# Expert steps of a token-routed kernel: gathered rows are turned in the middle of a step's low parts, each half of the next weights is loaded when its own buffer is free, and the state rows' ranks stand ahead of their gates

## What is computed

```python
def _moe_ref(x, w_in, w_out):            # 4352 rows of 512, hidden 2048
    h = x @ w_in
    g = np.maximum(0.01 * h, h)
    return g @ w_out

def _moe2_ref(x, w_gate, w_output_gate, w1, w2):     # 8 experts, hidden 1024
    logits = x @ w_gate
    e_idx = np.argmax(logits, axis=1)
    probs = softmax(logits);  gate_w = probs[arange(N), e_idx]
    eom = sigmoid(x @ w_output_gate)
    for e in range(E):
        mask = e_idx == e
        h = np.maximum(x[mask] @ w1[e], 0.0)
        out[mask] = gate_w[mask, None] * eom[mask, e, None] * (h @ w2[e])
```

## Time and profile before

| | us |
|---|---|
| median of 3 runs | 1158.08 |
| lowest and highest | 1157.42 and 1158.69 |
| the profiled execution | 1158.76 |
| its span in the trace | 1157.0 |
| PE busy | 1114.1 (96%) |
| DVE busy | 632.6 (55%) |
| ACT busy | 405.8 (35%) |
| POOL busy | 275.6 (24%) |

### The profile page before, as it was taken

One profiled execution on the slowest core, in us unless ns is written; L12 is line 12 of the kernel. 1 busy time (PEld: TensorE's weight loads), 2 busy tenths in 40 slices (PEclk: granted clock), 3 DMA queues, 4 the chain that ended last, 5 costly groups with the idle time before them and its releaser, 6 DMA issues.

```text
span 1157.0 us, 18341 instructions
## 1 busy us (share of the span) xinstructions
PE 1114.1 (96%) x6530; PEld 903.9 (78%) x6531; DVE 632.6 (55%) x1421; ACT 405.8 (35%) x754; POOL 275.6 (24%) x337
## 2 busy tenths in 40 slices
PE   5999999999999999999999999999999999888995
PEld 2777777777777777777777888889899989678884
DVE  6684574764854746747554577553433436366342
ACT  4344334434433443344343553321211214244211
POOL 1000001010010010000100203554455365655643
PEclk8999999999999999999999999999999999999998
DMA  9311120120210201200102411761111124443211
GB/s 346 125 45 37 37 78 1 42 73 1 76 40 18 80 19 37 79 1 1 37 1 75 126 38 48 201 195 55 39 48 59 37 56 98 144 105 107 55 39 35
DMA packets 41054, 79.01 MB, mean 68 GB/s; under 512 B 11398, under 2 KB 13190, under 8 KB 40967
## 3 DMA queue, kind: packets, MB, share of 16 engines
q1 hardware_dynamic: 29957, 53.48, 15.2%
q0 software_dynamic: 11040, 24.77, 7.5%
HBM read 60.31 MB, written 20.61 MB: 70 GB/s over the span
## 4 chain that ended last, share of the span: by engine, by line
PE 80%; DVE 6%; issue 4%; DMA 4%; POOL 2%; ACT 1%; POOLq 1%; SPq 0%; DVEq 0%; ACTq 0%
PE bank L529 25%; PE bank L531 24%; PE bank L530 24%; PE bank L562 3%; DMA raw<-w_dram 2%; POOL xq L438 2%; DMA xq<-rows_dram,part_now 2%; PE bank L580 1%; PE bank L596 1%; DVE w_lo L1338 1%; PE bank L604 1%; PE bank L540 1%; PE bank L569 1%; DVE g_buf L1213 0%; DVE o_buf L1600 0%
## 5 line engine op out<-in xcount | busy, mean ns | idle before, releaser
L529 PE MATMUL bank<-wout_lo,gT_hi 128*128 128x512 f32 x544 | 216.0, 397 | 0.0
L531 PE MATMUL bank<-wout_hi,gT_hi 128*128 128x512 f32 x544 | 212.7, 391 | 0.0
L530 PE MATMUL bank<-wout_hi,gT_lo 128*128 128x512 f32 x544 | 212.2, 390 | 0.0
L438 POOL DMA_INDIRECT xq<-rows_dram,part_now x160 | 170.5, 1066 | 69.4 <-issue 54.7
L423 POOL DMA_INDIRECT slots_dram<-tok_i,pos_i x34 | 34.4, 1010 | 616.3 <-DVE pos_i L1313 608.6
L1213 DVE TENSOR_TENSOR g_buf<-g_buf,bank 128x512 f32<-128x512 f32 (+1 forms) x144 | 94.3, 655 | 107.2 <-ACT g_buf L963 106.9
L529 PE MATMUL bank<-xgT_lo,w_hi 128*128 128x256 f32 x512 | 146.3, 286 | 6.0 <-DVE hT_lo L1469 4.7
L530 PE MATMUL bank<-xgT_hi,w_lo 128*128 128x256 f32 x512 | 145.6, 284 | 0.0
L531 PE MATMUL bank<-xgT_hi,w_hi 128*128 128x256 f32 x512 | 145.5, 284 | 0.0
L963 ACT ACTIVATE g_buf<-bank 128x512 f32<-128x512 f32 (+1 forms) x144 | 82.5, 573 | 151.7 <-PE bank L531 150.2
L1217 DVE TENSOR_TENSOR gT_lo<-g_buf,gT_hi 128x512 fp32r<-128x512 f32 (+1 forms) x144 | 95.4, 662 | 72.9 <-ACT gT_hi L969 71.4
(11 more groups left out here) (227 smaller groups left out, 1764.0 us busy)
## 6 DMA issues: line engine op xcount, KB each, us to landing
raw<-w_dram SPq DMA_DIRECT2D x20, 512.0 KB, 8.9
raw<-w_dram SPq DMA_DIRECT2D x10, 1024.0 KB, 14.5
rows_dram<-y_buf SPq DMA_DIRECT2D x8, 1032.0 KB, 4.5
X<-x_in_dram SPq DMA_DIRECT2D x8, 1024.0 KB, 5.5
XT<-xT_in_dram SPq DMA_DIRECT2D x7, 1024.0 KB, 5.7
win<-w_in_dram SPq DMA_DIRECT2D x4, 1024.0 KB, 11.6
y_buf<-w_out_dram POOLq DMA_DIRECT2D x6, 512.0 KB, 7.2
xq<-rows_dram,part_now POOLq DMA_INDIRECT x160
```

What stands on the lines that cost most here:

```text
L438: pool.indirect_dma_start(out=xq[:, 4 * u + a, :], out_offset=None, in_=quarters_dram, in_offset=bass.IndirectOffsetOnAxis(ap=part_now[:, ...
L529: pe.matmul(o, l_hi, r_lo, start=first, stop=False)
L530: pe.matmul(o, l_lo, r_hi, start=False, stop=False)
L531: return pe.matmul(o, l_hi, r_hi, start=False, stop=last)
```

## The change

Five edits.

1. In a step of two tiles DVE does `turn_quarters(i + 1)` behind `h_lo(i, 4)`, ahead of the last three.
2. SP loads `w1` of the next expert when pieces 0 to 3 of the last weights are split, and `w2` when all eight are.
3. The state rows' ranks on PE stand one `f` earlier; on DVE ranks and slots come ahead of the gates, of which only the sum stays in front.
4. `row_now` is written ahead of `plan_order`.
5. The eight stores of 32 state rows each become two of 128.

```diff
@@ SP
-            def load_expert(ex, between=None):
-                load_w1(ex)
-                if between is not None:
-                    sp.wait_ge(gathered, between)
-                load_w2(ex)
@@
             for t in range(2):
-                for q in range(4):
-                    first = (S + NS) * (4 * t + q) + S
-                    sp.dma_start(rows_dram[first:first + NS, :], y_buf[NS * q:NS * q + NS, t, :]).then_inc(y_stored, 16)
+                sp.dma_start(rows_dram.rearrange("(b s) n -> b s n", b=B)[4 * t:4 * t + 4, S:, :], y_buf[:, t, :]).then_inc(y_stored, 16)
@@ load_planned
+                w1_splits = 8 * v - DC if isinstance(v, int) else sp.snap(8 * v - DC)
                 with sp.If(c0 < c1):
                     sp.wait_ge(ctl_ready, 1)
+                    sp.wait_ge(e_lo_done, w1_splits)
+                    load_w1(expert)
+                    if between is not None:
+                        sp.wait_ge(gathered, between)
                     sp.wait_ge(e_lo_done, splits)
-                    load_expert(expert, between)
+                    load_w2(expert)
@@ POOL gather_step, and ACT ahead of its loop
-                pool.wait_ge(y_stored, 16 * (B + 8))
+                pool.wait_ge(y_stored, 16 * (B + 2))
@@ PE first_step_and_last_routing
                     if f == 2:
                         pe.wait_ge(lg_copied, B + 1)
-                    elif f == 3:
                         ranks(B, 2, rank_bank=oacc[0])
@@ DVE: route_gate loses its first instruction to sum_gates
+            def sum_gates(r, tiles):
+                step = Steps(dve, route_step, RS * r + 6, 1)
+                dve.wait_ge(edif_ready, r + 1)
+                step(dve.reduce_sum(gate[:, 0:T], edif[:, 0:T, :], AX.X))
@@ DVE, written-out stretch
             h_lo(0, 0)
-            route_gate(B, 2)
-            route_ranks(B, 2, rank_bank=oacc[0])
+            sum_gates(B, 2)
+            route_ranks(B, 2, rank_bank=oacc[0], after=7)
+            route_slots(B, 2, state=True, after=7)
             h_lo(0, 1)
-            route_slots(B, 2, state=True)
+            route_gate(B, 2, after=7 + 2 + 6)
             h_lo(0, 2)
@@
-            plan_order()
             dve.wait_ge(second_in, 16)
             dve.tensor_scalar(row_now[:, :], second_tok[:, :], NT - 1, None, ALU.min).then_inc(rows_copied, 2)
+            plan_order()
@@ DVE expert_step
                 if tiles == 2:
-                    for f in range(F2):
+                    for f in range(5):
                         h_lo(i, f)
                     turn_quarters(i + 1)
+                    for f in range(5, F2):
+                        h_lo(i, f)
```

More of the change, by code:

```diff
@@ L1096, in _ @@
             act.wait_ge(ctl_ready, 1)
-            act.wait_ge(y_stored, 16 * (B + 8))
+            act.wait_ge(y_stored, 16 * (B + 2))
             with act.Fori(0, E // 2) as w:
@@ L1262, in route, with route_gate @@
                 step.end()
-            def route_gate(r, tiles):
+            def sum_gates(r, tiles):
                 T = tiles
-                step = Steps(dve, route_step, RS * r + 6, 5)
+                step = Steps(dve, route_step, RS * r + 6, 1)
                 dve.wait_ge(edif_ready, r + 1)
                 step(dve.reduce_sum(gate[:, 0:T], edif[:, 0:T, :], AX.X))
+                step.end()
+            def route_gate(r, tiles, after=7):
+                T = tiles
+                step = Steps(dve, route_step, RS * r + after, 4)
                 step(dve.tensor_scalar(gate[:, 0:T], gate[:, 0:T], 1e-9, None, ALU.add))
@@ L1279, in route_gate, with route_ranks @@
                                   ez[:, 0:T].rearrange("p (t q n) -> p t q n", q=1, n=1).broadcast_to([P, T, DC, 1]), ALU.mult).then_inc(gate_ready, 1)
-            def route_ranks(r, tiles, rank_bank=aux[0]):
+            def route_ranks(r, tiles, rank_bank=aux[0], after=11):
                 T = tiles
                 dve.wait_ge(rank_ps, r + 1)
-                step = Steps(dve, route_step, RS * r + 11, T)
+                step = Steps(dve, route_step, RS * r + after, T)
                 for t in range(T):
@@ L1290, in route_ranks, with route_slots @@
                 step.end()
-            def route_slots(r, tiles, state=False):
+            def route_slots(r, tiles, state=False, after=11):
                 T = tiles
-                step = Steps(dve, route_step, RS * r + 11 + T, RS - 11 - T)
+                step = Steps(dve, route_step, RS * r + after + T, 6 if state else 7)
                 dve.wait_ge(rank_read, r + 2)
@@ L1316, in route_slots @@
                     step(dve.tensor_scalar(tokf[:, 0:T], tokf[:, 0:T], float(S + NS), None, ALU.add))
-                    step.end()
+                step.end()
             w8_row = const[0:1, C_W8:C_W8 + E]
@@ L1385, in layer @@
                         if f == 11:
+                            sum_gates(r, 4)
                             route_gate(r, 4)
```

## The result

| | us | |
|---|---|---|
| before | 1157.75 (1157.11 to 1158.69, 4 runs) | profiled execution 1158.76, span 1157.0 |
| after | 1167.16 (1165.79 to 1168.72, 4 runs) | profiled execution 1165.79, span 1164.0 |
| ratio | 1.0081, interval 1.0064 to 1.0098 | forecast 1156.3 (1152.0 to 1162.0) |

The changed kernel is slower by 0.8% on this chip. Sign and range of the forecast were wrong. The medians are 9.4 apart and the two traces 7.0: the profiled execution before was slower than its four timed ones, the one after was the fastest of its four.

What follows compares the result with a forecast made beforehand. PE, busy 80% of the span, was taken as the bound, changeable only through its gaps. Steps 1 and 2 with their lead +2.5, 11 to 14 -2.3, 15 to 18 -2.0: -1.8 in all, giving 1156.3 us (1152.0 to 1162.0).

Steps and rivals of the forecast that it cites:

- term of -2.07: PE's gap ahead of flip_rows(1), waiting for the rows of step 1: edits 3 and 4 remove it, -2.07 us.
- Rival C: Step 1's second gather isn't 2.3 earlier, as its stores or second_tok are late: +1.0, so 1157.3; chance 0.15.
- Edit 1 in step 1: Ahead of step 1's down part: PE waits 4.0 us for the gather, plus 1.6 of slow clock, together +5.6.
- Step 2: The gap of 1.00 at 759.17 goes, as step 2 starts later and w2 is issued earlier: -1.00 us.
- Step 11: Gather lands 3.3 us behind its last issue, at 954.8, so PE waits 1.0 (0.4 to 3.1).
- Step 12: Its gather starts 3 us earlier with only w1 ahead, landing at about 976: costs PE nothing.
- my own rule: In two-tile steps PE's down part can start no earlier than the gather's landing + 2.76 us.
- Steps 13 and 14: Step 13's gap of 2.43 goes and step 14's stays; together -3.3 us.
- Step 15: Gather lands at 1032.5 against a hidden part ending at 1033.5: PE waits 1.8 us, no clock loss.
- rival B: Step 15's gather waits behind both halves of the next weights: gap 6.7 plus clock 1.6, so 1162.8; chance 0.15.
- Step 16: Edit 2 lands the last expert's weights some 8 us earlier, removing a wait of 3.02 and 1.6 of slow clock: -4.6.
- rival A: Gathers land soon: step 1's gap 3.4 without clock loss, step 15's 0.8, so 1152.6; chance 0.21.

Runs made afterwards that it cites:

- chip D: The kernel before, unchanged, run on another chip for its trace there: 1168.82 us, ratio 1.0001.

## Why the prediction was wrong

**Edits 3 to 5: the step that failed first.** The term of -2.07 was right for edits 3 and 4 (-2.5 with eight stores). It failed at "this is hidden if two of 258 KB are no slower than one such": they were slower. Rival C had the right mechanism and the right place (the slots late, DVE held at `second_tok`, the plan late), but a chance of 0.15. Its sum is wrong too: it has the rows of step 1 about 1 later than before instead of 2.07 earlier, which is 3.1 more than the forecast and 1159.4, not +1.0 and 1157.3. The trace shows just that: +0.90 in step 0, 3.0 above the term, and `row_now` 3.6 later than with eight stores. The slots' scatter landed 7.4 behind its issue, at 718.0, as the two stores ended. I had 4 us for each store from 710.6 on, so their end at 718.6; the data moved from 712.2 to 718.4. So the 4 us were near, and the chance was too low.

**Edit 1 in step 1: right.** Gap 4.34 for 4.0. The down part behind it took 12.60 instead of 10.91, 1.69 of slow clock for 1.6; the last 0.16 of the 6.19 stand in the hidden part. Two errors cancelled, which is luck: the last gather issue was not at 737.2 but at 740.04 (the late plan), and step 1 itself started at 729.81, not 2.07 earlier. With eight stores, where neither happened, the gap was 4.12. The granted clock in the changed kernel:

```profile
740.00:744.00 4.00, 1.58 (x14) 1.38 (x12) 1.00 (x2) 1.00 (x3) 2.60 (x5) 1.00 0.27 75
744.00:748.00 4.00, 2.08 (x5) 1.70 (x6) 3.93 (x11) 3.99 (x6) 2.48 (x4) 0.75 0.82 215
748.00:752.00 4.00, 4.00 (x16) 3.20 (x16) 3.93 (x4) 0.72 (x1) 3.39 (x3) 0.82 1.03 405
```

**Step 2: right**, -1.26 for -1.00. But it was reckoned from the weights of before: with the turn last and the rows early, step 2 waits 3.29 for them. **Step 11: too much**, 0.16 for 1.0; the landing of 3.3 behind the last issue was a guess between 2.7 and 5.4, and the turn's wait was 0.60.

**Step 12: the wrong sentence** was "it lands at about 976, where it is wanted; nothing for PE, if it is late by 1 to 2 neither". 976 is 8.5 behind the step's start there; the turn started 11.2 behind it (983.93), 2.7 more. By my own rule, landing + 2.76 against a hidden part of 11.5, a landing late by 1 already costs. The last issue was at 976.44, and the rows landed 7.5 later, with both halves of the weights in flight (issued at 968.99 and 976.43), where I had only w1 ahead. +2.55. POOL's timeline and SP's queue there:

```profile
976.44 1.00 POOL L434 DMA_INDIRECT xq<-rows_dram,part_now  x1 [0.30 <-issue]
```
```profile
968.99 1.84 SPq L347 DMA_DIRECT2D raw<-w_dram  x4
976.43 0.94 SPq L351 DMA_DIRECT2D raw<-w_dram  x2
```

**Steps 13 and 14: right**, -2.92 and -0.81, together -3.73 for -3.3. Step 14's gap did not stay as it was: 0.81 of it went, and the wait ahead of step 15 took 1.57 more.

**Step 15: the term that was mis-sized most**, 1.8 against 7.71. The hidden part lasted 12.73, as taken (12.55). The rest was in the landing, 15.4 behind the step's start and not 11.55. It has two parts, in POOL's timeline and in SP's queue:

```profile
1030.56 1.95 POOL L434 DMA_INDIRECT xq<-rows_dram,part_now  x1 [0.30 <-issue]
1032.81 1.00 POOL L434 DMA_INDIRECT xq<-rows_dram,part_now  x1 [0.30 <-issue]
...
1035.43 1.01 POOL L434 DMA_INDIRECT xq<-rows_dram,part_now  x1 [0.30 <-issue]
```
```profile
1027.27 1.85 SPq L347 DMA_DIRECT2D raw<-w_dram  x4
1032.79 0.94 SPq L351 DMA_DIRECT2D raw<-w_dram  x2
```

First, the last issue came 8.2 behind the step's start instead of 6.9. In the kernel before three of the eight issues were long (1.95, 1.96, 1.78 for 1.00), now four in a row were (from 1023.70 to 1032.5). This part does not decide: with eight stores the last issue came 6.9 behind the start, as taken, and step 15 was still 31.04 long. Second, the rows landed 7.2 behind the last issue (7.6 with eight stores), not 4.7. w1 started with the step, as taken, but w2 followed 5.5 later at 1032.79, ahead of the last gather issues, where I had it behind. My 4.2 us had only what was left of w1 and the gathers' own bytes in front. This is rival B's mechanism, and its turning point of 6.5 was passed; I gave it 0.15 on the ground that w2 is issued "only about when the last gather is". That w2's bytes alone make the 2.5 was not tried. The granted clock:

```profile
1040.00:1044.00 4.00, 0.00 (x0) 0.00 (x0) 1.34 (x3) 0.96 (x2) 0.46 (x1) 0.87 1.03 351
1044.00:1048.00 4.00, 2.61 (x6) 2.13 (x7) 3.93 (x11) 3.99 (x6) 2.02 (x3) 0.50 0.66 224
```

Beside the gap of 5.42 the down part took 13.06 instead of 10.91, 2.15 of slow clock, where I had counted none.

**Step 16: right**, -4.76 for -4.6, but it was not edit 2's alone to give: with the loads together it is gone too, behind a longer step 15. **Step 18:** 0.10 for 0.8.

**The clock.** My rule, 1.6 for a gap of 3 us or more and nothing for a shorter one, is not borne out at its edge, and rival A did not keep to it (3.4, "too short for the clock"). Ahead of `flip_rows(1)` a gap of 2.96 in the changed kernel left the clock at 1.00, and gaps of 2.98 and 2.89 in two of its variants brought 0.57 and 0.50 in the stretch from 728 to 732, step 0 being 28.36 and 29.26 long instead of 26.92. With edit 1 alone a gap of 2.10 brought 0.59 there. One trace of each kernel can't price such a gap.

**The sum of the errors**: step 0 +3.0, step 15 +5.9, steps 12 to 14 +2.1, the rest -1.4; +9.6 on a forecast of -1.8 gives the +7.9 of the steps. The upper end of the range, 1162.0, was below rival B's own 1162.8. B's price for step 15 (+6.5) and C's as it should have been summed (+3.1) are both what came, and step 12 came on top. They were treated as alternatives, though both are late gathers or scatters behind other transfers. Rival D's sum is 0.2 off (1147.1 for 1147.3), which changes nothing.

## What to carry to other kernels

Before a consumer is moved ahead of work that hid its wait, write down for every step of that kind how far ahead of the new need its data lands; one landing taken for on time (12) and one lag reckoned with half of the traffic (15) decided the sign here. Count in what the later steps give back, too: a gap closed in one step (0) came back in another (2). Before merging DMA issues, look whether the new shape still spreads over the engines and whether something small and urgent follows it, as the slots' scatter did here. And take a gain of under 1% on more than one chip: here the same change is 1.0081 on one and 1.0009 on another.

## What the runs showed of the hardware

- Two stores of 258 KB, each into 4 blocks of rows, kept the 16 DMA engines 0.2 to 0.3 busy at some 93 GB/s for 6 us. A scatter issued behind them by POOL, on another queue, landed 7.4 later, against 2.3 to 2.6 in the same place beside eight stores of 32 rows.
- POOL's issue of an indirect gather takes 1.00, and mostly 1.95 to 2.03 while DVE's splits run (`w_lo<-raw,w_hi`, 1022.48 to 1029.4 and 1030.40 to 1032.8 in the changed kernel, beside four long issues from 1023.70 to 1032.5). The Trainium skill ("SBUF — State Buffer", section "SBUF: two separate sides") says that a VectorE instruction with two SBUF inputs contends with a GpSimd instruction that reads SBUF. The splits have two SBUF inputs; if the issue of a gather is such an instruction, the trace agrees in direction. That the issues would be quicker without the splits was not tried.
- Chips differ by 1% on this kernel, and where is visible: on three of four, PE issues its matmuls late in steps 1, 11 and 18, with gaps of up to 1.03 that nothing releases. In the kernel before on chip D that is 1.9 to 4.0 per step. None of the six traces of the faster kind has such a gap. Why these chips and these steps stays open; a trace names no releaser for them.
